# Nine gate logits by VectorE multiply-add passes over rows, in place of TensorE transposes and small matmuls

## The reference

```python
# 1: attention of 8 heads, local window and 32 global tokens        -> x   [4, 544, 512]
# 2: token-shifted feed-forward
xk = mu_k * x + (1.0 - mu_k) * x_prev
xr = mu_r * x + (1.0 - mu_r) * x_prev
k = np.maximum(xk @ w_k, 0.0)                                     # 512 -> 1024
v = k * k @ w_v                                                   # 1024 -> 512
x2 = 1.0 / (1.0 + np.exp(-(xr @ w_r))) * v
# 3: one of 8 experts for each token
logits = np.einsum('bsd,de->bse', x2, w_gate)                     # 8 numbers for each token
local_gate = 1.0 / (1.0 + np.exp(-np.einsum('bsd,de->bse', x2, w_local).squeeze(-1)))   # 1 more
# e = argmax(logits), or the expert of the token before, where local_gate >= 0.5
# out = softmax(logits)[e] * (np.maximum(x2 @ w1[e], 0.0) @ w2[e])
```

## Time and profile before

| what | us |
|---|---|
| median of three runs | 673.18 |
| the profiled execution | 674.25 |
| its span in the trace | 672.5 |
| attention ends, the keys of group 0 start | 121.4 |
| last value sums of group 4 done, last x2 starts | 382.4 |
| routing starts on VectorE | 387.3 |
| first matmul of the expert loop | 411.8 |

### The profile page before, as it was taken

The page is one execution under the profiler, slowest core; times in us unless marked ns, Lnnn a source line. Parts: engine busy times, 40 slices in busy tenths (PEclk is TensorE's granted clock), DMA queues, the critical chain, the costliest instruction groups (busy, mean ns, idle before and its releaser), DMA issues.

```text
span 672.5 us, 15064 instructions
## 1 busy us (share of the span) xinstructions
PE 639.7 (95%) x4662; PEld 531.8 (79%) x4663; DVE 356.2 (53%) x924; ACT 280.7 (42%) x615; POOL 160.3 (24%) x239
## 2 busy tenths in 40 slices
PE   7999999999999999999999928999999999999995
PEld 6888888777887887789889717887888888888883
DVE  3777789675355626444435684567253263263531
ACT  4777789345223512332423402475262162162521
POOL 3545556200000000000000002436234134134140
PEclk9999999999999999999999958999999999999998
DMA  8988882000100000010016152759345044054000
GB/s 328 324 270 299 274 289 54 1 1 16 48 1 0 32 31 0 0 47 17 0 60 239 59 222 76 251 187 327 95 147 178 31 173 165 31 169 160 11 19 10
DMA packets 30483, 78.08 MB, mean 116 GB/s; under 512 B 4330, under 2 KB 7146, under 8 KB 30448
## 3 DMA queue, kind: packets, MB, share of 16 engines
q1 hardware_dynamic: 24368, 63.47, 27.2%
q0 software_dynamic: 3200, 8.92, 3.8%
q10 hardware_dynamic: 2880, 5.24, 2.5%
HBM read 69.49 MB, written 9.70 MB: 118 GB/s over the span
## 4 chain that ended last, share of the span: by engine, by line
PE 89%; DVE 6%; issue 2%; ACT 1%; DMA 1%; POOL 1%; DVEq 0%; POOLq 0%; ACTq 0%
PE banks L724 23%; PE banks L726 22%; PE banks L725 22%; PE banks L600 3%; PE banks L887 3%; PE banks L667 2%; PE banks L758 2%; PE banks L676 2%; PE banks L630 1%; PE banks L861 1%; PE banks L614 1%; PE banks L750 1%; PE banks L644 1%; PE banks L640 1%; PE banks L691 1%
## 5 line engine op out<-in xcount | busy, mean ns | idle before, releaser
L1351 DVE TENSOR_SCALAR hid<-banks 128x512 f32<-128x512 f32 x40 | 27.6, 691 | 94.2 <-PE banks L726 92.7
L1378 ACT ACTIVATE prob<-neg,negmax 128x160 f32<-128x160 f32 (+1 forms) x136 | 59.1, 436 | 29.4 <-DVE negmax L946 19.8
L724 PE MATMUL banks<-we,hid_hi 128*128 x160 | 66.8, 417 | 1.4 <-DVE hid_lo L1356 1.4
L1467 ACT ACTIVATE we<-we_raw 128x1024 f32 (+1 forms) x64 | 63.1, 1051 | 7.8 <-issue 7.8
L724 PE MATMUL banks<-we,xg_hi 128*128 x160 | 65.2, 408 | 0.0
L725 PE MATMUL banks<-we,xg_hi 128*128 x160 | 63.2, 395 | 0.0
L1107 DVE TENSOR_TENSOR we<-we_raw,we 128x1024 f32 (+1 forms) x50 | 60.8, 1258 | 4.4 <-PEq L787 4.4
L726 PE MATMUL banks<-we,xg_lo 128*128 x160 | 63.1, 394 | 0.0
L726 PE MATMUL banks<-we,hid_lo 128*128 x160 | 63.0, 394 | 0.0
L725 PE MATMUL banks<-we,hid_hi 128*128 x160 | 63.0, 394 | 0.0
L528 POOL MEMSET xg<- 128x1024 f32 x1 | 1.0, 952 | 258.9 <-PE banks L726 258.9
(11 more groups left out here) (220 smaller groups left out, 1383.2 us busy)
## 6 DMA issues: line engine op xcount, KB each, us to landing
we_raw<-in_w_e SPq DMA_DIRECT2D x64, 512.0 KB, 4.5
qk<-in_qk_t SPq DMA_DIRECT2D x32, 448.0 KB, 6.3
vw<-in_v_t SPq DMA_DIRECT2D x32, 256.0 KB, 4.9
w_raw<-in_w_mix ACTq DMA_DIRECT2D x20, 256.0 KB, 4.6
x_rows<-x SPq DMA_DIRECT2D x17, 256.0 KB, 2.0
vz<-in_v_z SPq DMA_DIRECT2D x8, 128.0 KB, 4.0
vx<-in_v_x SPq DMA_DIRECT2D x8, 96.0 KB, 5.5
qg<-in_qg_t SPq DMA_DIRECT2D x8, 64.0 KB, 7.3
```

Source lines behind the costliest of these rows:

```text
L724: pe.matmul(dst, left[0], right[0], start=first, stop=False)
L1351: dve.tensor_scalar(hid[:, D * h:D * (h + 1)], ps_h[:, h, :], 0.0, None, ALU.max).then_inc(hid_ready, 1)
L1378: act.activation(prob[:, t % 2, c], neg[:, c], ACT.Exp, scale=-1.0, bias=negmax[:, t % 2, k:k + 1], accum_out=rsum[:, t % 2, k:k + 1]).the ...
L1467: act.activation(we_hi[:, buf, 2 * j:2 * j + 2, :].rearrange("p x a b -> p x (a b)"), we_raw[:, j, :].unsqueeze(1), ACT.Copy).then_inc(we_ ...
```

## The change

The nine logits move from TensorE to VectorE. For each tile nine `tensor_tensor_reduce` passes multiply the 128 rows of `x2` (token on partitions, 512 features along the row) by one column of the weights, which the host hands over repeated on all 128 partitions, and add up along the row. The product itself goes to PSUM banks 6 and 7 in turn and is not read. Eight of the nine weight rows are loaded over those columns of `xT` that groups 0 and 1 have used up; SyncE starts that load when the inputs of group 1 are made. Before its first pass VectorE waits for it. The passes of a group's last tile are dealt out one to each key part of the next group. Gone are the transposes, ScalarE's copies of turned tiles, the small matmuls, `x2t` and `w9`.

With it come these moves: squares are rounded by ScalarE and no longer by VectorE; both inputs of the next group are made before the first `x2` of a group; of the first expert's weights parts 0 to 3 go to other places in SBUF and part 4 on is loaded only when the last keys are done, the second expert's load starts behind the last logit, the rests of parts 4 and 5 are taken after the routing by VectorE, and of 6 and 7 by GpSimd; `by_gate` waits for the second gather's indices (`rows_in_ready`), not for the first gather's issue.

```diff
-        w9 = sb("w9", [P, DC, E + 1])
+        dot = sb("dot", [P, 2, E + 1])
...
+        def w9(e):
+
+            return w9_last[:] if e == E else xT[:, e // 2, D * (e % 2):D * (e % 2 + 1)]
...
+            sp.wait_ge(mix_added, 2 * DC * 2)
+            for c in range(E // 2):
+                sp.dma_start(xT[:, c, 0:2 * D], w_9[:, 2 * D * c:2 * D * (c + 1)]).then_inc(w9_loaded, 16)
+            sp.dma_start(w9_last[:], w_9[:, D * E:D * (E + 1)]).then_inc(w9_loaded, 16)
...
-                    if t >= 1:
-                        turn_x2(n0 + t - 1, parity(n0, t - 1))
-                    if t >= 2:
-                        logits(n0 + t - 2, parity(n0, t - 2))
...
+            def dots(n, par, es=range(E + 1)):
+
+                for e in es:
+                    if e == 0:
+                        dve.wait_ge(x2_ready, n + 3)
+                    if e >= 2 or not (isinstance(n, int) and n == 0):
+                        dve.wait_ge(dotted, (E + 1) * n + e - 1)
+                    dve.tensor_tensor_reduce(product[:, e % 2, :], x2[:, par, :], w9(e), 1.0, 0.0, ALU.mult, ALU.add,
+                                             dot[:, par, e:e + 1]).then_inc(dotted, 1)
+                    if e == E:
+                        dve.wait_ge(dotted, (E + 1) * (n + 1))
+                        dve.tensor_copy(logit[:, bass.ds(n, 1), :], dot[:, par, :]).then_inc(logit_ready, 1)
...
-                    dve.wait_ge(k_squared, n + 3)
-                    dve.tensor_copy(k2_hi[:, f, 0:w], raw).then_inc(k2_hi_ready, 1)
...
+                    if not first_group(g):
+                        dots(n0 - 1, parity(n0, -1), range(f, f + 1) if f < FC - 1 else range(f, E + 1))
+                    if f > 0:
+                        rest_of_squares(f - 1)
...
                     mix_inputs(g + 1, 0, tiles_after)
+                    mix_inputs(g + 1, 1, tiles_after)
...
+                    if first_group(g) and t == 0:
+                        dve.wait_ge(w9_loaded, 16 * (E // 2 + 1))
+                    if t < tiles - 1:
+                        dots(n, parity(n0, t))
...
-            dve.wait_ge(rows_asked, 1)
+
+            dve.wait_ge(rows_in_ready, 2)
...
+                def round_squares(f):
+                    act.wait_ge(k_squared, FC * g + f + 3)
+                    act.activation(k2_hi[:, f, 0:w], k2_raw[:, f % 2, 0:w], ACT.Copy).then_inc(k2_hi_ready, 1)
```

More of the change, by code:

```diff
@@ L375, in _ @@
                 load_values(0, i)
-            for dst, src in ((muT, mu), (w9, w_9)):
-                sp.dma_start(dst[:], src).then_inc(consts_loaded, 16)
+            sp.dma_start(muT[:], mu).then_inc(consts_loaded, 16)
             for b in range(1, B):
@@ L401, in _ @@
             for j in range(PARTS):
-                sp.dma_start(we_raw[:, j, :], w_e[j * P:(j + 1) * P]).then_inc(we_loaded[j], 16)
+                if j == PARTS // 2:
+                    sp.wait_ge(mix_used[0], GROUPS)
+                sp.dma_start(raw_part(0, j), w_e[j * P:(j + 1) * P]).then_inc(we_loaded[j], 16)
             for n in range(early, NT):
                 store(n, n % 2)
-            with sp.Fori(1, E) as e:
+            sp.wait_ge(logit_ready, NT)
+            sp.wait_ge(we_lo_ready, VPARTS + PARTS // 2)
+            sp.wait_ge(we_hi_ready, PARTS)
+            for j in range(PARTS):
+                sp.dma_start(we_raw[:, j, :], w_e[(PARTS + j) * P:(PARTS + j + 1) * P]).then_inc(we_loaded[j], 16)
+            with sp.Fori(2, E) as e:
                 for j in range(PARTS):
@@ L542, in _ @@
             gather(0, 0)
-            pool.sem_inc(rows_asked, 1)
             gather(1, 1)
+            for j in range(VPARTS, PARTS):
+                pool.wait_ge(we_hi_ready, j + 1)
+                rest_of_part(0, slice(0, 1), j).then_inc(we_last_lo_ready, 1)
             pool.wait_ge(tables_ready, 1)
@@ L743, in _ @@
             keys_part(0, GT, 1)
-            def turn_x2(n, par):
-                pe.wait_ge(x2_ready, n + 3)
-                pe.wait_ge(x2t_ready, n + 1)
-                for c in range(DC):
-                    mm = pe.transpose(ps_x[:, P * c:P * (c + 1)], x2[:, par, P * c:P * (c + 1)], ident[:])
-                mm.then_inc(x2_turned, 1)
-            def logits(n, par):
-                pe.wait_ge(x2t_ready, n + 2)
-                pe.wait_ge(logit_ready, n + 2)
-                for c in range(DC):
-                    mm = pe.matmul(ps_l[:, 0:E + 1], x2t[:, par, P * c:P * (c + 1)], w9[:, c, :],
-                                   start=(c == 0), stop=(c == DC - 1))
-                mm.then_inc(logit_summed, 1)
             def mix_group(g, tiles):
@@ L771, in mix_group @@
                     keys_part(g, tiles, f)
-                    if f < 2 and not first_group(g):
-                        if f == 0:
-                            turn_x2(n0 - 1, parity(n0, -1))
-                        logits(n0 - 2 + f, parity(n0, f))
                 pe.drain().then_inc(mix_used[0], 1)
@@ L1145, in _ @@
                 mix_group(g, SIZES[g], SIZES[g + 1] if g + 1 < GROUPS else 0)
-            for n in range(NT - 2, NT):
-                keep_logits(n)
+            dots(NT - 1, (NT - 1) % 2)
             steps = [0]
@@ L1320, in _ @@
             ins.then_inc(gate_onehots_ready, 1)
+            first_weights(range(PARTS // 2, VPARTS))
             ps_h, ps_ht, ps_g = banks[:, 0:2, :], banks[:, 2:4, :], banks[:, 5, :]
@@ L1492, in mix_group @@
                     act.activation(recept[:, t % (GT - 1), :], ps_r[:, parity(n0, t), :], ACT.Sigmoid).then_inc(r_ready, 1)
-                    if t == 1 and tiles_after:
-                        mix_inputs(g + 1, 0, tiles_after)
-                if tiles_after:
-                    mix_inputs(g + 1, 1, tiles_after)
-                else:
+                    if t < 2 and tiles_after:
+                        mix_inputs(g + 1, 0, tiles_after, range(0, 2) if t == 0 else range(2, DC + 1))
+                    if t == GT - 2 and tiles_after:
+                        mix_inputs(g + 1, 1, tiles_after)
+                if not tiles_after:
                     rounded_weights(0, slice(0, 1), range(3, PARTS))
-                for t in range(tiles - 1):
-                    keep_turned(n0 + t, parity(n0, t))
             mix_group(0, GT, GT)
```

101 lines of the change are left out of this document (43 added, 58 removed).

## The result

The change made the kernel slower: 684.42 us median against 673.19 beside it on the same chip, a ratio of 1.0161 (95% interval 1.0137 to 1.0185). The profiled execution took 683.06, where the forecast said 671.0. It is slower by 1.6%, and clear of the noise.

A forecast was written before the change was run, and what follows sets the result against it. TensorE, 89% of the chain that ended last, was taken as the bound. Against 674.25 profiled: -20.0 - 0.6 + 7.2 + 6.2 + 2.6 + 1.7 - 0.3 gave 671.0 profiled, 670.0 median; range 665.5 to 675.5.

The forecast's parts named there:

- the first expert's rests, put at 0: After the routing: two rests on VectorE at 1.1 us each, done before the loop's first matmul; 0, 1 at most.
- the pass of 0.61: VectorE's logit passes: each 512-column pass holds the queue 0.61 us, between 0.56 and 0.69.
- Off TensorE, -20.0 and -0.6: Logits of 15 tiles leave TensorE's path at 1.33 us each, -20.0; squares in group 0's keys go to ScalarE, -0.6.
- The first rival: A pass costs over 0.64 us, so the gain is gone; at 0.69, 679.4 us; chance 12%.
- The wait for the weights, +6.2: Group 0: passes wait for w9's load of 8 us, and TensorE's fourth value tile waits 6.2 us for the second x2.
- The third key parts, +7.2: TensorE waits for the first square at third key parts: 2.5, 2.5, 1.3, 0.7, plus 0.2 at one fourth value tile.
- The tail, +2.6: Before the routing: the last x2 starts 1.0 us late and its passes reach the routing 1.6 later, +2.6.
- The clock, +1.7: TensorE's clock may fall at the waits of 2.5 and 1.3 us, unrecovered: 0, 1.7 or 3.4; 1.7 taken.
- by_gate, -0.3: First gathers: by_gate starts behind the second copy of indices, no longer beside the first gather's issue; -0.3 us, 0 to -0.5.
- the rival of 732 us: A pass runs at half rate, 1.14 us, with two SBUF inputs and a sum; about 732 us; chance 5%.

The follow-up runs named there:

- the squares' edit alone: The kernel before with only the squares changed: ScalarE rounds them, VectorE takes their rests one part later; 672.28 us, ratio 0.9983.
- all four edits: Changed kernel with every second product in SBUF, late rests behind the gathered tile, logit weights loaded in halves, passes spread; 660.57 us, ratio 0.9798 to the kernel before.
- the fewer passes between: On top of all four edits, fewer passes between the products of groups 0 and 1, the others two a key part; 656.33 us, ratio 0.9744 to the kernel before.
- the late rests: Changed kernel with VectorE's two rests (parts 4 and 5) moved behind the gathered tile's rest and the gate's sum; 679.45 us, ratio 1.0086 to the kernel before.
- the extra matmuls: Kernel with the late rests and every second product in SBUF, plus 22 unread matmuls in TensorE's wait in group 0; 675.25 us against 674.6 without them.
- the order alone: Changed kernel with the same passes spread, eight between two products, the rest among key parts; 674.31 us, ratio 1.0013 to the kernel before.

## Why the prediction was wrong

It said 670.0 and faster, at 0.67; it is 684.4 and slower. Two steps failed: the first expert's rests, put at 0, cost 6.3 us, and the pass of 0.61 cost 0.65, some 3.5 us. Up to the routing the places of gain and loss held, and the layout was some tenths short in each group; behind the routing the path itself was wrong.

- **Off TensorE, -20.0 and -0.6**: right. Where nothing waits the four stretches lose 20.6 us, and the keys of group 0 lose 0.75 in the changed kernel and 0.76 with the squares' edit alone.
- **The pass at 0.61**: it is 0.65 back to back, since each pass into PSUM follows another into PSUM. The passes in the trace of before were 160 columns wide and wrote their product to `neg`, not to a PSUM bank, so they could not show it. Its price by the forecast's own factor is 117 x 0.038 = 4.4 (seven steps from 174.39 to 178.93, 0.648 each); measured were 3.8 by the runs and 3.45 by the landmarks. The first rival ("over 0.64") named it at 12%, for another reason (the write-out and the waits of nine sums in a row); by its arithmetic 0.65 alone would have given 670.0 + 4.4 = 674.4, close to no change and not 11 us slower.
- **The first expert's rests at 0, "1 at most"**: the largest miss, 6.3 us (34.5 to 28.2). The sum took 1.1 us a rest from columns, and alone they take that (1.16), but it forgot whose company they have. It also asked whether they are done before the loop's matmul, and not what stands behind them on VectorE: the rest of the gathered tile, for which TensorE waits.
- **The wait for the weights, +6.2**: right in size (6.09). The first pass came 28.3 us behind the landmark, where the layout had 27.5: the load was issued 0.5 later and took 0.3 longer. With every second product in SBUF the first pass came 28.6 behind it, 1.1 late, and group 0 is 1.2 us over (65.77 for 64.6); that the one is the other was not tested.
- **The third key parts, +7.2**: right in place; with 0.61 a pass (the run with every second product in SBUF) groups 1 to 3 and the stretch to the routing lie 0.75, 0.4, 0.55 and 0.3 over the forecast's layout, for which the cause was not looked for. The changed kernel's are larger by the pass.
- **The tail, +2.6**: 2.7 with all four edits, with and without the fewer passes between, where a pass is 0.61; 3.4 in the changed kernel.
- **The clock, +1.7**: a fall costs 1.6 us of a group, as the forecast had it. But it is not the same in all executions: the profiled one of the changed kernel had neither the one at 250 nor the one at 310, that of the late rests had both. The fall at 180 costs nothing, as the forecast argued and the extra matmuls showed.
- **by_gate, -0.3**: it started 1.7 us later counted from the routing, and cost nothing. The first gather's issue did take 1.25 for 1.58, but the rounding of the first gathered tile starts 22.7 us behind the routing's start in both kernels, so the -0.3 did not come.

The sum put right by the landmarks, against 674.25: -4.6, + 3.45 for the pass, + 3.15 that the layout is short at 0.61, + 6.45 behind the routing, + 0.15 ahead of the first landmark (the keys of group 0 0.15 shorter than forecast, their start 0.3 later): +8.6, 682.9. Measured were 683.06. This is bookkeeping on the traces, and the 3.15 is what was left over in it; it proves no term.

What the forecast didn't ask was whether its own +7.2 had to be. The layout that gave it has VectorE busy for 1.8 of 2.72 us in a key part (the trace shows it idle for 0.8 to 1.4 from the third on), and TensorE waiting ahead of the third. Both stood in the same working.

## What to carry to other kernels

Work moved from the bounding engine to a free one is worth its whole time only when the free engine's queue lets the bounding one go: lay the added work out in quanta, put what frees a buffer first, and put the rest into the idle places. Here the order alone was worth 10 us, and 8.8 on top of the other edits. An operation moved to another place is priced by what stands behind it on its queue and by which other engine works on the same memory at the time, not by its columns alone. And a rule that one has just applied to one pair of engines is to be run over all other pairs in the change.

## What the runs showed of the hardware

- Two passes in a row with a sum, both with products of 512 columns into PSUM: 0.65 us apart. Every second one into SBUF: 0.61 for both. The write-out of the sum takes 0.14 behind a PSUM product and 0.08 behind one in SBUF, and lies beside the next pass in both.
- Two SBUF inputs and a sum over 512 columns don't run at half rate in this instruction: 0.61 us, where the rival of 732 us had 1.14. The Trainium skill (Vector Engine (DVE) Microarchitecture Reference, section 7, points that are easy to get wrong) states half throughput for a scalar-tensor-tensor form with two non-bf16 SBUF sources. The pass is another instruction (`CUSTOM_DVE_ANT_0` in the trace), so its rule does not carry over to it, and no run here tests the form that it names.
- VectorE's subtraction of two SBUF inputs over 1024 columns: 1.16 us each alone, 7.40 for two while GpSimd does two of its own in 4.65. All of the loss is VectorE's: its first took 6.26, and GpSimd's took 2.36 and 2.34 beside it and 2.36 without it.
- TensorE's granted clock after a wait of 3.05 us: kept at 1.00 in one execution, down to 0.50 for about 3 us in another, with an identical program up to there. Such a fall cost 1.6 us.
